# Three more weight pieces loaded during the last attention item, and a third of the slot inputs moved between the logits, in a fused attention, soft-MoE and top-1-MoE kernel

## What is computed

```python
logits = x @ phi                                  # 3072 tokens x 32 slots
d = softmax of logits over the tokens             # one column per slot
slot_input = (d.T @ x).reshape(8, 4, 512)         # 8 experts, 4 slots each
for e in range(8):
    slot_out[e] = np.maximum(slot_input[e] @ w1[e], 0) @ w2[e]
c = softmax of logits over the slots              # one row per token
return c @ slot_out
```

## Time and profile before

| | |
|---|---|
| median of 3 runs | 440.69 us (439.51 to 441.41) |
| the profiled execution | 439.07 us |
| its span, first to last instruction | 437.4 us |
| TensorE busy | 421.4 us (96%) |
| VectorE, ScalarE, GpSimd busy | 239.2, 212.2, 210.0 us |
| moved by DMA | 89.21 MB, mean 204 GB/s |

### The profile page before, as it was taken

One profiled execution on the slowest core, in us unless ns is written; L12 is line 12 of the kernel. 1 busy time (PEld: TensorE's weight loads), 2 busy tenths in 40 slices (PEclk: granted clock), 3 DMA queues, 4 the chain that ended last, 5 costly groups with the idle time before them and its releaser, 6 DMA issues.

```text
span 437.4 us, 9412 instructions
## 1 busy us (share of the span) xinstructions
PE 421.4 (96%) x3036; PEld 353.6 (81%) x3037; DVE 239.2 (55%) x791; ACT 212.2 (49%) x418; POOL 210.0 (48%) x216
## 2 busy tenths in 40 slices
PE   8999999999999999998797999999999999999996
PEld 7899999999999997743234977688888888888884
DVE  6667777777767775556100679574333323333344
ACT  3887788788888773422010016373333333332244
POOL 5899999999999910010001020234333344443422
PEclk9999999999999999999999999999999999999999
DMA  7866989898977304999995488511111111112111
GB/s 236 278 220 251 402 345 393 343 364 317 393 262 240 106 21 133 391 391 409 397 386 211 140 294 289 217 55 60 60 53 43 60 60 60 60 36 58 55 54 14
DMA packets 29174, 89.21 MB, mean 204 GB/s; under 512 B 3440, under 2 KB 6000, under 8 KB 29136
## 3 DMA queue, kind: packets, MB, share of 16 engines
q1 hardware_dynamic: 25456, 78.47, 48.4%
q0 software_dynamic: 3360, 9.83, 7.2%
q10 hardware_dynamic: 320, 0.42, 0.4%
HBM read 80.85 MB, written 8.13 MB: 203 GB/s over the span
## 4 chain that ended last, share of the span: by engine, by line
PE 85%; DMA 7%; DVE 3%; issue 2%; ACT 1%; POOL 0%; SPq 0%; ACTq 0%; DVEq 0%; POOLq 0%
PE O L445 17%; PE Yq L1626 11%; PE Yq L1627 10%; PE Yq L1628 10%; PE PT L427 9%; PE S L418 5%; PE S L417 5%; DMA ext<-in_moe_w 5%; PE Gp L1557 3%; DMA w2h<-in_moe_w 2%; PE XTp L893 2%; PE Lp L982 2%; PE Cp L1529 2%; PE O L395 2%; PE Up L902 1%
## 5 line engine op out<-in xcount | busy, mean ns | idle before, releaser
L523 ACT ACTIVATE shared<-shared,nm 128x256 f32<-128x256 f32 (+1 forms) x192 | 83.7, 484 | 30.3 <-DVE nm L636 30.1
L445 PE MATMUL O<-V,PTs 128*128 128x65 f32 x704 | 90.1, 269 | 0.0
L636 DVE CUSTOM_DVE_ANT_0 shared<-S,TA 128x256 f32<-128x256 f32 (+1 forms) x192 | 68.7, 396 | 34.4 <-PE S L418 31.7
L445 PEld LDWEIGHTS O<-V,PTs 128*128 128x128 f32 x704 | 86.5, 191 | 1.1 <-issue 1.0
L1626 PE MATMUL Yq<-w2h,hh 128*128 x208 | 83.0, 399 | 0.4 <-issue 0.4
L1627 PE MATMUL Yq<-w2l,hh 128*128 x208 | 81.2, 390 | 0.0
L1628 PE MATMUL Yq<-w2h,hl 128*128 x208 | 81.2, 390 | 0.0
L380 POOL TENSOR_TENSOR kl<-k_raw,kh 128x816 fp32r<-128x816 f32 x30 | 57.9, 1931 | 5.0 <-ACT kh L538 2.9
L1913 DVE SCALAR_TENSOR_TENSOR hl<-Gp,hh 128x512 fp32r<-128x512 f32 x56 | 38.1, 688 | 39.4 <-ACT hh L1724 39.4
L376 POOL TENSOR_TENSOR qs<-q_raw,qs 64x768 fp32r<-64x768 f32 x30 | 54.7, 1825 | 2.4
L427 PE MATMUL PT<-ident,shared 128*128 128x128 f32 x352 | 54.7, 274 | 0.0
(11 more groups left out here) (248 smaller groups left out, 571.7 us busy)
## 6 DMA issues: line engine op xcount, KB each, us to landing
mem<-in_moe_w SPq DMA_DIRECT2D x9, 2048.0 KB, 11.6
ext<-in_moe_w SPq DMA_DIRECT2D x6, 2048.0 KB, 19.8
V<-in_v SPq DMA_DIRECT2D x16, 715.0 KB, 6.8
k_raw<-in_k SPq DMA_DIRECT2D x13, 816.0 KB, 7.0
q_raw<-in_q SPq DMA_DIRECT2D x13, 768.0 KB, 4.6
xmem<-in_moe_w SPq DMA_DIRECT2D x2, 2048.0 KB, 11.1
w2h<-in_moe_w SPq DMA_DIRECT2D x1, 2048.0 KB, 10.2
w2l<-in_moe_w SPq DMA_DIRECT2D x1, 2048.0 KB, 15.5
```

The source lines that it names most:

```text
L445: mm = pe.matmul(O[grp % 2][:, at:at + VC], PTs[:, par, (h * kbs + kb) * P:(h * kbs + kb + 1) * P], V[:, buf, h, vb, :], start=(n == 0), s ...
L523: nc.scalar.activation(Pb[:, par, h, 0:width(g)], Pb[:, par, h, 0:width(g)], ACT.Exp, bias=nm[:, par, h:h + 1], scale=-1.0).then_inc(exp_d ...
L636: v.tensor_tensor_reduce(Pb[:, par, h, 0:w], S[par][h][:, 0:w], tab, -SCALE, HUGE, ALU.add, ALU.min, nm[:, par, h:h + 1]).then_inc(biased, 1)
```

## The change

A constant `EARLY` = 3 is new. Three pieces (4, 5 and 6) are now loaded into `ext` while item 15 runs. For that `qs`, `kh`, `kl` and `V` are laid out as a buffer for each parity, the four even ones side by side with a small filler behind each `V`, so that the first three slots of `ext` lie over `q_raw`, `k_raw` and the even buffers only. Each load waits for its part of these: piece 4 for the last split of q and k, piece 5 for the last scores of item 14, piece 6 for the last weighing of item 14. Piece 7 is the first that waits for `x_turned`. The ring keeps its 10 slots.

The slot inputs of tiles 0 to 7 move into the loop, between `logits(5)` and step 7. `largest(0)` and `turn_back(0)` move ahead of `logits(4)`, ScalarE's `lt_copy(0)` and `exps(0)` and VectorE's `shift(0)` move ahead by one copy each. Behind the loop four tiles of the first set are left ahead of `largest(1)`, `busy(2)` becomes `busy(4)`, and the 8 idle products ahead of piece 14 go.

```diff
@@ -50,6 +50,7 @@
 WSIZE = DC * F
 MEMW = 4
 EXT = 8 - MEMW
+EARLY = 3
 XSLOTS = TT * D // WSIZE
 NSLOT = MEMW + EXT + XSLOTS - 1
 
@@ -91,6 +92,10 @@
                     sb(ctx, "lt", [P, P])]
         xst = ExitStack()
         xmem = sb(xst, "xmem", [P, XSLOTS, WSIZE])
+
+        place = ExitStack()
+        ext = sb(place, "ext", [P, EXT, WSIZE])
+        place.close()
         X = xmem[:].rearrange("p a (t d) -> p (a t) d", d=D)
 
         sp_passed = sem("sp_passed")
@@ -138,13 +143,18 @@
 
 
     st = ExitStack()
+
 
     q_raw = sb(st, "q_raw", [P, 2, 2, SEQ])
     k_raw = sb(st, "k_raw", [P, 2, 2, QT * KSLOT])
-    qs = sb(st, "qs", [P, 2, 2, SEQ], F32R)
-    kh = sb(st, "kh", [P, 2, 2, QT * KSLOT], F32R)
-    kl = sb(st, "kl", [P, 2, 2, QT * KSLOT], F32R)
-    V = sb(st, "V", [P, 2, 2, VB, VC])
+    qs, kh, kl, V = [], [], [], []
+    for buf in range(2):
+        qs.append(sb(st, f"qs{buf}", [P, 2, SEQ], F32R))
+        kh.append(sb(st, f"kh{buf}", [P, 2, QT * KSLOT], F32R))
+        kl.append(sb(st, f"kl{buf}", [P, 2, QT * KSLOT], F32R))
+        V.append(sb(st, f"V{buf}", [P, 2, VB, VC]))
+
+        sb(st, f"V{buf}_end", [P, 8])
     nin = sb(st, "nin", [P, 4], I32)
     nf = sb(st, "nf", [P, 8])
     nw = sb(st, "nw", [P, 2, 2])
@@ -251,7 +261,7 @@
 
     def load_v(sp, item, buf):
 
-        sp.dma_start(V[:, buf].rearrange("p h b c -> p (h b c)"), v_d[item]
+        sp.dma_start(V[buf][:].rearrange("p h b c -> p (h b c)"), v_d[item]
                      ).then_inc(v_loaded[buf], 16)
 
     @block.sync
@@ -295,6 +305,15 @@
                     sp.wait_ge(head_table, HEADS - 2)
                 if item % 2 and 5 <= item < 5 + 2 * MEMW:
                     load_piece(sp, (item - 5) // 2, mem[:, (item - 5) // 2, :])
+
+            sp.wait_ge(q_split, parts(ITEMS - 1))
+            sp.wait_ge(k_split, parts(ITEMS - 1))
+            load_piece(sp, MEMW, ext[:, 0, :])
+
+            sp.wait_ge(qk_done, (ITEMS - 1) * QT)
+            load_piece(sp, MEMW + 1, ext[:, 1, :])
+            sp.wait_ge(pv_done, (ITEMS - 1) * QT)
+            load_piece(sp, MEMW + 2, ext[:, 2, :])
         with sp.Else():
             sp.dma_start(phi_sb[:], phi_d.rearrange("(c p) s -> p c s", p=P)).then_inc(small_loaded, 16)
             sp.dma_start(wg_sb[:], wg_d.rearrange("(c p) s -> p c s", p=P)).then_inc(small_loaded, 16)
@@ -311,6 +330,8 @@
             sp.wait_ge(d_normed, ITEMS + 2)
             for i in range(MEMW):
                 load_piece(sp, i, mem[:, i, :])
+            for i in range(EARLY):
+                load_piece(sp, MEMW + i, ext[:, i, :])
 
     @block.gpsimd
     def _(pool):
@@ -368,17 +389,17 @@
-                    nc.gpsimd.tensor_copy(qs[:, buf, :, cq], q_raw[:, buf, :, cq]).then_inc(q_high, 1)
+                    nc.gpsimd.tensor_copy(qs[buf][:, :, cq], q_raw[:, buf, :, cq]).then_inc(q_high, 1)
...
@@ -755,7 +776,7 @@
     TW = QT4 * P
     QUADS = SETT // 4
     EG = NE // REP
-    ext = sb(st, "ext", [P, EXT, WSIZE])
+    sb(st, "ext_place", [P, EXT, WSIZE])
     XL = sb(st, "XL", [P, TT * P])
     C4 = XL[:].rearrange("p (t r s) -> p t r s", r=4, s=SLOTS)
     XT = XL[:].rearrange("p (b n) -> p b n", b=2)
@@ -849,7 +870,7 @@
     def _(sp):
 
         sp.wait_ge(x_turned, 1)
-        for i in range(MEMW, len(PIECES)):
+        for i in range(MEMW + EARLY, len(PIECES)):
             if i >= MEMW + EXT and i < NSLOT:
 
                 sp.wait_ge(si_parts, i - MEMW - EXT + 1)
@@ -936,7 +957,7 @@
 
         def here(i):
 
-            if i >= len(PIECES) - 2:
+            if i >= len(PIECES) - 1:
 
                 busy(8, STp)
             pe.wait_ge(slot_loaded[i % NSLOT], 16 * (i // NSLOT + 1))
@@ -997,21 +1018,23 @@
             for k in range(2 * DC):
                 for q in range(QUADS):
                     turn(k, q)
-                if k >= 1:
-                    logits(k - 1)
                 if k == DC + 1:
                     largest(0)
                     turn_back(0)
+                if k >= 1:
+                    logits(k - 1)
+                if k == 2 * DC - 2:
+
+                    inputs(range(0, TT // XSLOTS))
             logits(2 * DC - 1)
 
             for n in range(2 * DC * QUADS - len(XTp), 2 * DC * QUADS):
                 pe.wait_ge(*copied(n))
 
-            inputs(range(0, REP))
+            inputs(range(TT // XSLOTS, SETT))
             largest(1)
             turn_back(1)
-            inputs(range(REP, SETT))
-            busy(2)
+            busy(4)
             inputs(range(SETT, TT))
             pe.wait_ge(dsum_done, 1)
             pe.matmul(Mp[:, P:P + SLOTS], ones[:], dsum[:], start=True, stop=True).then_inc(dtot_done, 1)
@@ -1071,10 +1094,10 @@
                                  ACT.Exp).then_inc(d_exp2, 1)
 
         for n in range(1, 2 * DC * QUADS, 2):
-            copy_group(act, nc.scalar.copy, n)
             if n == (DC + 1) * QUADS:
                 lt_copy(0)
-            if n == (DC + 3) * QUADS:
+            copy_group(act, nc.scalar.copy, n)
+            if n == (DC + 3) * QUADS - 2:
                 exps(0)
         lt_copy(1)
         exps(1)
@@ -1156,7 +1179,7 @@
             copy_group(dve, v.tensor_copy, i)
             if i == (DC + 1) * QUADS - 1:
                 largest(0)
-            if i == (DC + 2) * QUADS:
+            if i == (DC + 2) * QUADS - 2:
                 shift(0)
         sum_up(0)
         largest(1)
```

More of the change, by code:

```diff
@@ L121, in build @@
         attended = sem("attended")
-        attend = attention(nc, ctx, sb, psum, sem, block, attended, mem, X, shared, ident, ones, Rsel, phi_sb, wg_sb, load_piece,
+        attend = attention(nc, ctx, sb, psum, sem, block, attended, mem, ext, X, shared, ident, ones, Rsel, phi_sb, wg_sb, load_piece,
                   sp_passed, const_ready, rsel_ready, small_loaded, q_d, k_d, v_d, n_d, phi_d, wg_d)
-        soft_moe(nc, ctx, sb, psum, sem, block, attend, attended, mem, xmem, X, ident, ones, Rsel, phi_sb, load_piece,
+        soft_moe(nc, ctx, sb, psum, sem, block, attend, attended, mem, ext, xmem, X, ident, ones, Rsel, phi_sb, load_piece,
                  slot_loaded, rsel_ready, small_loaded, STR, Cn, CT, c_stored, st_out, ct_out, counting, r_iota, lt_done, c_dram)
@@ L129, in build, with attention @@
         both.close()
-def attention(nc, ctx, sb, psum, sem, block, attended, mem, X, shared, ident, ones, Rsel, phi_sb, wg_sb, load_piece,
+def attention(nc, ctx, sb, psum, sem, block, attended, mem, ext, X, shared, ident, ones, Rsel, phi_sb, wg_sb, load_piece,
               sp_passed, const_ready, rsel_ready, small_loaded, q_d, k_d, v_d, n_d, phi_d, wg_d):
@@ L375, in _ @@
                         pool.wait_ge(k_split, done)
-                    nc.gpsimd.tensor_tensor(qs[HD:P, buf, :, cq], q_raw[HD:P, buf, :, cq],
-                                            qs[HD:P, buf, :, cq].bitcast(F32), ALU.subtract).then_inc(q_split, 1)
+                    nc.gpsimd.tensor_tensor(qs[buf][HD:P, :, cq], q_raw[HD:P, buf, :, cq],
+                                            qs[buf][HD:P, :, cq].bitcast(F32), ALU.subtract).then_inc(q_split, 1)
                     pool.wait_ge(q_split, done + 1)
                     pool.wait_ge(k_high, 2 * item - 1 + p if halves else 2 * item)
-                    nc.gpsimd.tensor_tensor(kl[:, buf, :, ck], k_raw[:, buf, :, ck],
-                                            kh[:, buf, :, ck].bitcast(F32), ALU.subtract).then_inc(k_split, 1)
+                    nc.gpsimd.tensor_tensor(kl[buf][:, :, ck], k_raw[:, buf, :, ck],
+                                            kh[buf][:, :, ck].bitcast(F32), ALU.subtract).then_inc(k_split, 1)
         with pool.Else():
@@ L415, in scores @@
                 else:
-                    q = qs[:, buf, h, t * P:(t + 1) * P]
-                    pe.matmul(S[par][h][:, 0:w], q, kh[:, buf, h, at:at + w], start=True, stop=False)
-                    mm = pe.matmul(S[par][h][:, 0:w], q, kl[:, buf, h, at:at + w], start=False, stop=True)
+                    q = qs[buf][:, h, t * P:(t + 1) * P]
+                    pe.matmul(S[par][h][:, 0:w], q, kh[buf][:, h, at:at + w], start=True, stop=False)
+                    mm = pe.matmul(S[par][h][:, 0:w], q, kl[buf][:, h, at:at + w], start=False, stop=True)
             mm.then_inc(qk_done, 1)
@@ L445, in weigh @@
                     mm = pe.matmul(O[grp % 2][:, at:at + VC], PTs[:, par, (h * kbs + kb) * P:(h * kbs + kb + 1) * P],
-                                   V[:, buf, h, vb, :], start=(n == 0), stop=(n == len(blocks) - 1))
+                                   V[buf][:, h, vb, :], start=(n == 0), stop=(n == len(blocks) - 1))
             mm.then_inc(pv_done, 1)
@@ L496, in general @@
                             mm = pe.matmul(O[h][:, t * VC:(t + 1) * VC], PTd[:, kb * P:(kb + 1) * P],
-                                           V[:, 0, h, kb, :], start=(kb == 0), stop=(kb == QT - 1))
+                                           V[0][:, h, kb, :], start=(kb == 0), stop=(kb == QT - 1))
```

(6 more changed lines are left out.)

## The result

The changed kernel takes 444.06 us as the median of 6 runs (442.61 to 445.51), the kernel before 439.79 us. The ratio is 1.0094 with a 95% interval of 1.0071 to 1.0118. The forecast was 439.2 us with a range that ended at 441.8, so the kernel is slower, by 4 us, where a gain of 1.5 us was expected. The profiled execution took 445.38 us over a span of 443.7 us.

The account below looks back on a forecast made before the run. Piece 15's landing was taken to bound the first MoE. Piece 10's landing saves 2.2 us, the moved products lose 0.7: 1.5 us gained, 440.69 - 1.5 = 439.2 us, range 437.0 to 441.8.

Parts of the forecast that it names:

- the cost of the early loads: Attention: loading pieces 4 to 6 early costs nothing, as items take 9.85 us at 331 and at 82 GB/s.
- The gap of 2.87 us: First MoE, TensorE's gap called issue ahead of hidden(1): keeps its 2.87 us and only moves by 0.7.
- the term that the prediction was about: Weight stream after hidden(0): early loads shorten piece 10's landing by 2.2 us; piece 15 lands at 235.9 instead of 237.40.
- 12 pieces to 9 is not 16 us: Weight stage: taking 3 of 12 pieces out looks like 16 us less, but the ring's second condition prevents that.
- the ring: Weight slots: piece 10 needs piece 0's slot, so six pieces start after hidden(0) begins; only queueing ahead of piece 10 is saved.
- the bound of the prediction in which piece 9 masks its start: Piece 10's landing: piece 9 lands at 203.2, piece 10 one 5.1 us transfer later, at 208.3; 2.6 us gained.
- the case that it took for the sum: Piece 10 meets almost no queue and lands 9.4 us after issue, at 209.4 instead of 210.87; 1.5 us gained.
- 26.7 by the rates: From piece 10's landing to piece 15's: one w1 piece and four w2 pieces without a gap, 26.7 us; 26.5 measured before.
- Rival D: First MoE: waits for pieces 14 and 15 with fewer idle products drop the clock to 1.2 GHz; +2.3, 443.0 us; chance 0.06.
- costed at nothing: First MoE: the 8 idle products removed ahead of piece 14 had filled a wait, so removal costs nothing.
- The inputs moved between the logits: After logits(5): these products add 1.81 us; their wait for exps(0) is zero or some tenths.
- the working: Behind the loop: busy(4) ends at 192.67, second-set inputs need exps(1) at 192.74; hidden(0) and piece 10's issue 0.7 us late.

Follow-up runs that it names:

- run 1: Changed kernel with the order of TensorE, ScalarE and VectorE put back, 8 idle products included; layout and three early loads stay: 444.43 us against 439.75 before, ratio 1.0105.
- run 3: Changed kernel with one early piece (EARLY = 1) instead of three: 439.61 us against 439.75 for the kernel before, ratio 0.9992.
- run 6: Kernel before, with two unneeded 2 MB memory-to-memory transfers issued at 158 us: 444.70 us against 440.06, ratio 1.0098.
- run 7: Changed kernel with pieces 5 and 6 held back until VectorE has passed its branch: 439.56 us against 440.06 for the kernel before, ratio 0.9979.
- run 4: Changed kernel with 12 idle products added ahead of TensorE's wait for VectorE's first copy: 442.48 us against 439.75 for the kernel before, ratio 1.0046.
- run 2: Changed kernel with all moves but no early load (EARLY = 0): 439.93 us against 439.75 for the kernel before, ratio 1.0009.
- run 8: One early piece in the order of the kernel before: 439.61 us against 440.06 for the kernel before, ratio 1.0002.
- run 10: Two early pieces in the order of the kernel before: 439.93 us, ratio 0.9996 to the kernel before.
- run 5: Changed kernel with two early pieces (EARLY = 2) instead of three: 438.05 us against 440.06 for the kernel before, ratio 0.9972.
- run 9: Changed kernel with two early pieces and the moves, measured again with more rounds: 439.39 us against 440.02 for the kernel before, ratio 0.9979.

## Why the prediction was wrong

**The step that failed** is the cost of the early loads, "So nothing". It was argued from attention items with and without traffic, and for the items it holds: the attention's last normalisation on VectorE before the branch is 0.15 us later in the changed kernel. But between the items and the first MoE there is VectorE's branch, and its fetch ran in engines that stood empty ahead of 169 us (and the quarter from 167.25 above). With the loads in them the branch took 3.0 us longer. The empty engines were read as room for weights, not as the cover of something else. The rows were at hand: VectorE's gap of 2.75 us in the chain at 166.51, and the two queues of kind instruction on the page. The gap of 2.87 us was even used in the sum, as a constant; it came out as 3.62.

**What it cost**, from the start of `hidden(0)`, 5.37 us late in the profiled runs: 0.15 for the attention's end; 3.0 for the longer gap (2.95 in the chain, 5.70 - 2.75); 1.5 for the half clock behind it (the 8 transposes 1.97 instead of 1.09, the 8 logits products 1.44 instead of 0.78); 0.7 for the moved products. The sum is 5.35. Runs 1, 3, 6 and 7 show the second term, run 4 the third (in one profile), run 2 the fourth.

**What came back** is the term that the prediction was about. From `hidden(0)`'s start to piece 15's landing it was 237.40 - 197.28 = 40.1 us before. After, piece 15 is issued at 220.5 and lands 20.0 us later, 240.5 - 202.65 = 37.9. The forecast was 235.9 - 198.0 = 37.9. This distance holds over the profiles: 39.8 with the moves alone (run 2), 39.0 with early loads in the old order (runs 1, 8 and 10), and 37.8 to 38.0 with both (after, runs 3, 4, 5, 7 and 9). So "12 pieces to 9 is not 16 us" was right: the ring lets through 2.2 us, half of it for the loads alone, half more with the moves, which cost 0.7 in `front`.

That the total is right to 0.1 us is luck, as two of its terms were off in opposite directions. Piece 10 landed 7.9 us after its issue and not 9.4, 5.1 us behind piece 9: that is the bound of the prediction in which piece 9 masks its start (8.3 us), not the case that it took for the sum. And a w1 piece that met engines at 0.00 took less than the 9.4: piece 8 landed 7.8 us after its issue. Piece 15 landed 28.0 us behind piece 10 and not 26.5, against 26.7 by the rates. Part of that is a dip where w1 ends: in run 5 the engines moved 305 and 215 GB/s in the two microseconds from 212, in the kernel before 412 and 377, which makes about 0.7 us, an estimate from these four numbers. What makes the dip and the rest is open.

**What was then added.** TensorE met its own branch at 219.78. That gap was 3.62 us instead of 2.87. Queue 8's packet of kind instruction started 0.99 us into it, against 0.13 us before, and in all twelve profiles TensorE went on 1.7 us behind the end of that packet. The clock fell behind the gap: 64 instructions of `hidden(1)` took 9.69 us, against 7.07 for the same number at full clock. TensorE, not the landing, then set the start of the last products: those of piece 14 ended at 239.69, the 8 idle ones at 241.67, 1.2 us behind the landing. The landing was 3.1 us late, so the last products started 4.2 us late. The other 2.1 us of the span lie in the second MoE, where the clock fell at 249 and 273. No code there was changed.

**The clock over the runs.** The changed kernel's six runs have mean clocks from 0.981 to 0.995 and times of 442.61 us (0.995) to 445.38 (0.981) and 445.51 (0.985). Runs of the kernel before with 1.000 took 438.7 to 439.8, one with 0.982 took 443.5. Whether the clock falls behind TensorE's branch isn't told by the length of that gap: in the profiles it fell behind 2.83 us (run 1), 2.88 us (runs 6 and 8) and 3.05 to 3.62 us (after, runs 3, 4, 7, 9 and 10), but not behind 2.87 (before), 2.92 (run 2) or 3.27 (run 5). Runs 5 and 9 are one kernel, and it kept its clock behind 3.27 us and lost it behind 3.22. Rival D had the clock in the right stage, but for the waits on pieces 14 and 15; in the changed kernel it was the branches. Why it fell at 249 and 273 stays open.

**Other steps.** Taking away the 8 idle products ahead of piece 14 was costed at nothing. In the changed kernel no wait is left there, so it took 2.0 us out of TensorE's work (run 1 still has them, at 235.62 in its chain); in run 2 the wait is there without them and the clock falls, as told there. The inputs moved between the logits didn't wait for `exps(0)`: in the chain they follow `logits(5)` directly (188.49 + 0.78 = 189.27), and `exps(0)` had ended at 189.10. The inputs of the second set did wait for `exps(1)`, 0.51 us where the working has 0.07.

## What to carry to other kernels

Idle DMA engines beside a branch may be the cover of a code fetch: before moving loads into such a place, look for the queues of kind instruction and for gaps called issue, and price each of them as it would be under full traffic (here 3 us). Hold the loads back until the engine has passed its branch, or size them so that they have drained by then; one or two pieces did, three didn't. And where a ring of slots feeds the transfers, ask which condition holds the last piece before counting the bytes saved.

## What the runs showed of the hardware that was not expected

VectorE took 2.9 to 3.6 us from start to start across its branch when the DMA engines were idle or draining (before, runs 2, 3, 5 and 7 to 10), and 5.8 to 6.4 us when they were full, whether with weights into SBUF (after, runs 1 and 4) or with copies from memory to memory (run 6). The packet of queue 14 began 0.5 to 1.0 us behind the end of VectorE's last operation in the first case and 3.2 to 3.7 us in the second. TensorE's gap at its branch, always under full traffic, was 2.8 to 3.6 us. A w1 transfer of 2.10 MB that met engines at a DMA share of 0.00 landed 7.6 to 8.1 us after its issue (piece 8 of the changed kernel and of runs 5, 9 and 10), against 9.7 us for the first one of w2 in the earlier trace rows.
